# Finished outputs of a convolution and two FFN layers: turned on DVE in 32x32 blocks and stored in runs of 128 bytes, instead of turned on PE

## The chip, the cores and the metric

The kernel runs on one core of a Trainium2 chip. The metric is the device time of one execution, in microseconds; lower is better. The engines are PE (TensorE, matrix products), DVE (VectorE), ACT (ScalarE), POOL (GpSimd) and SP (SyncE, which here only issues DMAs). They run side by side and wait for each other through semaphores.

## What is computed

```python
# x [2, 4096, 192]; weight_gen [2, 4096, 8 heads, 7 taps]
w = softmax(weight_gen, axis=-1)
x_pad = six rows of zeros ahead of x          # a causal window of 7 tokens
out[b, s, h, :] = sum_k w[b, s, h, k] * x_pad[b, s + k, h, :]     # 24 channels per head
x = out.reshape(8192, 192)
h = x @ w_in;   g = np.maximum(0.01 * h, h);  x = g @ w_out       # 192 -> 2048 -> 192
h = x @ w_in2;  r = np.maximum(h, 0.0);       return (r * r) @ w_out2
```

All of it is in float32. Each product is made from a high and a low part of both operands ("hi" and "lo"), as three matmuls.

## The kernel before

The 8192 tokens are split into 16 chunks (`NCH`) of 512 tokens: partition p holds tokens 64p to 64p + 63, and a chunk is 4 of these per partition (`TPC`). A chunk passes two layers, so there are 32 segments (`SEGS`): segment s works on one layer (`LAYER[s]`) of one chunk (`CHUNK[s]`). The layers alternate: segments 0 and 1 are layer 0 (of chunks 0 and 1), then even segments are layer 1 and odd ones layer 0, and 30 and 31 are both layer 1. In the steady part one period is an even segment and an odd one.

A segment has 8 steps (`PR`). On PE, `up(s, j)` multiplies 256 of the 2048 hidden rows into one of two PSUM pairs (`hb`, "h_pair" in the profile), and `down(s, j)` multiplies the activated result into the accumulators `ym` and `yr`. Between them ACT and DVE make the high and low part of the activation: in layer 0 ACT writes both the high part and `g` from PSUM and DVE subtracts (`gate_lo`, writes "g_lo"); in layer 1 ACT writes `u`, DVE `g` (`gate_of`), ACT the high part (`gate_hi`), and DVE the low part. `down` runs about two steps behind `up`; `steps_of` writes the order out by hand: for a segment up 0, the last two downs of the segment before around up 1, then up 2, up 3, down 0, up 4, down 1, up 5, down 2, a turn, down 3, up 6, down 4, up 7, down 5. (In segments 0 and 2 the turn stands later.) No engine reorders anything: each works through its own list and waits for semaphores.

`up` and the turns take the two PSUM pairs by turns (`made`, `PAIR`), and each waits until the one two before it has been read (`pair_free`).

PE holds activations channel by token, while the input and output rows are token by channel. So there is a turn in each segment: before an odd segment `turn_x` transposes the next chunk's convolution, and in an odd segment s of 3 to 31 `turn_y` transposes the outputs of layer 1 that the segment before has finished. Those outputs take this way: ACT copies half of the accumulators (`fold` on ACT), DVE adds the other half (`fold`, at j = 1, and `fold_end`, at j = 2) into `y_main` (128 channels) and `y_rest` (the other 64), both in the tile "raw_w_in"; PE turns them with 12 transposes against an identity into a PSUM pair; ACT copies them from there into `y_tok` (`y_out`, at j = 5); SP stores `y_tok` with one DMA (`store`). DVE also does the convolution for the next chunk in slices between its other work (`conv_ops`, `IN_UP`, `IN_DOWN`). SP's list in the steady part is: wait for the convolution, load the next x window and tap logits, wait for the finished outputs, store. The very last chunk has its own end (`last_out`, `last_fold`, `last_turn`), which writes the same `y_tok` after it has waited for the stores of all earlier chunks.

Of the kernel before, what the change touches and what calls it, by code (L numbers as in the profile page):

```python
# [5 lines left out]
def conv_two_ffn_kernel(nc, x, wgen, w_in1, w_out1, w_in2, w_out2, out):  # L6
    fp32 = mybir.dt.float32
    fp32r = mybir.dt.float32r
    ALU = mybir.AluOpType
# [7 lines left out]
    P = 128  # L17
# [35 lines left out]


    NEXT_X = [CHUNK[s + 1] if s + 1 < SEGS and LAYER[s + 1] == 0 else None for s in range(SEGS)]
    Y_OUT = [CHUNK[s - 1] if s and LAYER[s - 1] == 1 else None for s in range(SEGS)]
    assert not any(a is not None and b is not None for a, b in zip(NEXT_X, Y_OUT))

    LATE_TURNS = (0, 2)

    def steps_of(s):


        turn = [("turn", s)] if NEXT_X[s] is not None or Y_OUT[s] is not None else []
        early, late = ([], turn) if s in LATE_TURNS else (turn, [])
        if s == 0:
            return ([("up", 0), ("up", 1), ("up", 2), ("down", 0), ("up", 3), ("down", 1), ("up", 4), ("down", 2), ("up", 5)]
                    + early + [("down", 3), ("up", 6), ("down", 4)] + late + [("up", 7), ("down", 5)])
        before = [[("down", -2)], [("down", -1)]]
# [14 lines left out]
    PAIR[("last turn",)] = len(made) % 2  # L84
    made.append(("last turn",))
    TURNS = [m for m in made if m[0] != "up"]

    SOFT = 6
    TAPS = 2 * K - 1
# [23 lines left out]
    with ctx:  # L113
# [55 lines left out]
        y_tok = raw_in[1][:, :, :].rearrange("p a c -> p (a c)").rearrange("p (t d) -> p t d", d=D)  # L169
        ident = sb("identity", [P, HP])  # L170


# [47 lines left out]
        y_free = sem("y_banks_free")  # L220
        y_summed = sem("y_rest_summed")
        y_taken = sem("y_taken")
        y_turned = sem("y_transposed")
        turned_taken = sem("transposed_pair_taken")

        last_rest_done = sem("last_y_rest_done")
# [13 lines left out]
        def _(sync):  # L240
# [56 lines left out]

            def store(c):

                if c < NCH - 1:  # L300
                    sync.wait_ge(turned_taken, TURNS.index(("turn", c * 2 + 3 if c < NCH - 2 else SEGS - 1)) + 1)
                else:
                    sync.wait_ge(last_out_act, 2)
                    sync.wait_ge(last_out_dve, 1)
# [21 lines left out]
            for c in range(NCH):  # L326
                if c + 3 < NCH:

                    sync.wait_ge(conv_op, before(c + 3))
                    load_chunk(c + 3)  # L330
                store(c)
            sync.wait_ge(stored, 16 * NCH)

        @block.gpsimd
        def _(pool):
# [13 lines left out]
        def _(act):  # L349
# [60 lines left out]
                act.activation(fold_main[:, :], ym[0][:, :], ACT.Copy).then_inc(half_out, 1)  # L410
                act.activation(fold_rest[:, :], yr[0][:, :], ACT.Copy).then_inc(half_out, 1)

            def y_out(c, pair):
                act.wait_ge(y_turned, c + 1)
                if c:

                    act.wait_ge(stored, 16 * c)
                act.activation(y_tok[:, :, 0:P].rearrange("p t (a d) -> p a t d", a=2),
                               hb[pair][:, :, 0:QC].rearrange("p a (t d) -> p a t d", d=HP), ACT.Copy)
                act.activation(y_tok[:, :, P:D].rearrange("p (a t) d -> p a t d", a=2),  # L420
                               hb[pair][:, :, QC:QC + P].rearrange("p a (t d) -> p a t d", d=REST),
                               ACT.Copy).then_inc(turned_taken, 1)

            def up_out(s, j):
                n = s * PR + j
                pair = PAIR[("up", n)]
# [26 lines left out]
            def last_out():  # L453
                act.wait_ge(last_rest_done, 1)
                act.activation(fold_rest[:, :], yr[0][:, :], ACT.Copy).then_inc(last_rest_copied, 1)
                act.wait_ge(down_done, SEGS * PR)
                act.activation(fold_main[:, :], ym[0][:, :], ACT.Copy).then_inc(last_main_copied, 1)

                act.wait_ge(stored, 16 * (NCH - 1))
# [3 lines left out]
                act.wait_ge(y_turned, NCH)  # L463
                act.activation(y_tok[:, :, 0:HP], hb[PAIR[("last turn",)]][:, 0, 0:QC].rearrange("p (t d) -> p t d", d=HP),
                               ACT.Copy).then_inc(last_out_act, 1)

            def segment(s):
                for j in range(PR):
# [39 lines left out]
                    if NEXT_X[s] is not None and j == (6 if s in LATE_TURNS else 5):  # L508
# [4 lines left out]
                    if Y_OUT[s] is not None and j == 5:  # L513
                        y_out(Y_OUT[s], PAIR[("turn", s)])
# [21 lines left out]
        def _(dve):  # L536
# [153 lines left out]
            def fold(s):  # L690
                dve.wait_ge(half_out, s * 2 + 1)

                if LAYER[:s + 2].count(1):
                    dve.wait_ge(staged_taken, LAYER[:s + 2].count(1))
                if LAYER[s] == 0:
                    dve.tensor_tensor(stage[:, :], ym[1][:, :], fold_main[:, :], ALU.add)
                else:

                    dve.tensor_tensor(y_main[:, :].rearrange("p (t a c) -> p a t c", a=2, c=HP),  # L699
                                      *(t.rearrange("p (a t c) -> p a t c", a=2, c=HP)  # L700
                                        for t in (ym[1][:, :], fold_main[:, :])), ALU.add)
                dve.wait_ge(half_out, s * 2 + 2)
                upper = fold_rest[REST:P, :]
                dve.tensor_tensor(fold_sum[:, :], yr[1][0:REST, :], fold_rest[0:REST, :], ALU.add).then_inc(y_summed, 1)  # L704
                dve.tensor_tensor(upper, yr[1][REST:P, :], upper, ALU.add).then_inc(y_free, 1)  # L705

            def fold_end(s):
# [3 lines left out]
                if LAYER[s] == 0:  # L711
                    dve.tensor_tensor(stage_rest[:, :], fold_sum[:, :], upper, ALU.add).then_inc(y_taken, 1)
                else:
                    one, two = (t.rearrange("p (a h t c) -> p h a t c", a=2, h=2, c=HP) for t in (fold_sum[:, :], upper))
                    for h in range(2):
                        last = dve.tensor_tensor(
                            y_rest[h * REST:(h + 1) * REST, :].rearrange("p (t a c) -> p a t c", a=2, c=HP),
                            one[:, h, :, :, :], two[:, h, :, :, :], ALU.add)
                    last.then_inc(y_taken, 1)

            def gate_of(s, j):
                n = s * PR + j
# [58 lines left out]
            def last_fold():  # L781
# [10 lines left out]
                dve.wait_ge(stored, 16 * (NCH - 1))  # L792
                dve.wait_ge(y_turned, NCH)
                dve.tensor_copy(y_tok[:, :, HP:P], hb[PAIR[("last turn",)]][:, 1, 0:QC].rearrange("p (t d) -> p t d", d=HP)
                                ).then_inc(last_out_dve, 1)

            def segment(s):
                for j in range(PR):
# [5 lines left out]
                        fold(s - 1)  # L804
                    if s and j == 2:
                        fold_end(s - 1)
                    if s == 0 and j == 5:
                        first_segment(j)
                    if s == 1:
# [62 lines left out]
        def _(pe):  # L872
# [59 lines left out]
                                            conv_rest[r, t, :, :].rearrange("p h d -> p (h d)"), ident[r, :])  # L932
                last.then_inc(x_turned, 1)

            def turn_y(s, key):

                pe.wait_ge(y_taken, s + 1)
                pair_free(key)
                h = hb[PAIR[key]]
                for t in range(TPC):  # L940
                    for i, r in enumerate(ROWS):
                        pe.transpose(h[:, i, t * HP:(t + 1) * HP], y_main[r, t * P:(t + 1) * P], ident[r, :])  # L942
                for t in range(TPC // 2):
# [101 lines left out]
            def last_turn():  # L1045
# [18 lines left out]
                last.then_inc(y_turned, 1)  # L1064

            turn_first()
            for s in range(SEGS):
                for what, j in steps_of(s):
# [8 lines left out]
                            down(s, j)  # L1077
                    elif s == 0:
                        turn_second(("turn", s))
                    elif NEXT_X[s] is not None:  # L1080
                        turn_x(NEXT_X[s], ("turn", s))
                    else:
                        turn_y(s - 1, ("turn", s))
            down(SEGS - 1, PR - 2)
            last_down()
            last_turn()
# [20 lines left out]
```

## Time and profile before

| | |
|---|---|
| median of 3 runs | 1139.68 us (1139.62 to 1139.77) |
| profiled execution | 1142.64 us |
| its span in the trace | 1140.9 us |
| PE busy | 1132.4 us (99%), granted clock 1.0 throughout |
| DVE busy | 854.9 us (75%) |
| ACT busy | 667.4 us (59%) |
| hardware DMA queue | 15280 packets, 30.14 MB |

The profile is of one execution. Its span runs from the first to the last instruction; the time of the execution includes what lies around it. Busy times are the time in which an engine had at least one instruction under way. In the trace a matmul's line is that of the helper that issues it: L963 is `up`, L1008 and L1012 are `down`, L942 and L945 `turn_y`, L928 and L931 `turn_x`.

### The profile page before, as it was taken

To read this page: it belongs to the slowest core of one execution; us is meant where nothing else is said; L and a number is where in the kernel's file an instruction comes from. 1 tells how busy PE (TensorE), PEld (TensorE's weight loads), DVE (VectorE), ACT (ScalarE), POOL (GpSimd) and SP (SyncE) were. 2 spreads that over 40 slices of the span, in tenths; PEclk is the share of its full clock that TensorE was granted. 3 is DMA by queue.
4 is the path that set the end of the run, shared out by engine and by line. 5 is a ranking of instruction groups with operands and counts; after the bars stand their busy time and mean duration, and the time that the engine had idled before them with its cause. 6 is when DMAs were issued, how large, how long until landed. Compare 5 with 4: busy or idle time off the path is not lost.

```text
span 1140.9 us, 22894 instructions
## 1 busy us (share of the span) xinstructions
PE 1132.4 (99%) x10276; PEld 1115.3 (98%) x10276; DVE 854.9 (75%) x1036; ACT 667.4 (59%) x815; POOL 3.8 (0%) x11
## 2 busy tenths in 40 slices
PE   8999999999999999999999999999999999999998
PEld 6899999999999999999999999999999999999998
DVE  7888776877768787687877878777687776874574
ACT  4665656566565665656556556555656656566564
POOL 1000000000000000000000000000000000000000
PEclk9999999999999999999999999999999999999999
DMA  7311001010000101001010010100101001000000
GB/s 176 107 57 40 1 15 40 15 40 13 8 35 15 40 15 40 1 15 40 15 40 1 15 40 15 40 1 15 40 15 40 1 15 40 15 1 15 1 1 28
DMA packets 15378, 31.60 MB, mean 28 GB/s; under 512 B 1590, under 2 KB 10932, under 8 KB 15280
## 3 DMA queue, kind: packets, MB, share of 16 engines
q1 hardware_dynamic: 15280, 30.14, 8.2%
q8 instruction: 80, 1.31, 0.5%
q14 instruction: 18, 0.15, 0.0%
HBM read 23.84 MB, written 6.29 MB: 26 GB/s over the span
## 4 chain that ended last, share of the span: by engine, by line
PE 96%; DVE 1%; DMA 1%; ACT 1%; SPq 0%; issue 0%; DVEq 0%
PE h_pair L963 45%; PE y_main_psum L1008 30%; PE y_rest_psum L1012 20%; DMA x_window<-in_x_dram 1%; DVE tap_product L577 0%; PE h_pair L942 0%; PE h_pair L928 0%; PE h_pair L897 0%; DMA raw_w_in<-in_moe_w_in_dram 0%; DVE g_lo L737 0%; SPq L284 0%; DVE u L614 0%; ACT g_hi L429 0%; ACT g L433 0%; ACT w_in_parts L353 0%
## 5 line engine op out<-in xcount | busy, mean ns | idle before, releaser
L963 PE MATMUL h_pair<-x_parts,w_in_parts 64*128 64x512 f32 x4590 | 568.3, 386 | 0.5 <-issue 0.4
L963 PEld LDWEIGHTS h_pair<-x_parts,w_in_parts 64*128 64x128 f32 x4590 | 518.1, 184 | 5.9 <-issue 0.8
L1008 PE MATMUL y_main_psum<-g_hi,w_out_parts 64*128 64x512 f32 x2040 | 451.3, 389 | 0.0
L737 DVE TENSOR_TENSOR g_lo<-g,g_hi 128x1024 fp32r<-128x1024 f32 x255 | 311.5, 1222 | 141.0 <-ACT g_hi L441 87.0
L1008 PEld LDWEIGHTS y_main_psum<-g_hi,w_out_parts 64*128 64x128 f32 x2040 | 242.6, 184 | 2.1 <-issue 0.2
L441 ACT ACTIVATE g_hi<-g 128x1024 fp32r<-128x1024 f32 x127 | 134.8, 1062 | 170.6 <-DVE g L728 170.6
L429 ACT ACTIVATE g_hi<-h_pair 128x1024 fp32r<-128x1024 f32 x128 | 131.7, 1029 | 175.5 <-PE h_pair L963 175.4
L1012 PE MATMUL y_rest_psum<-g_lo,w_out_parts 64*128 64x512 f32 x1020 | 224.6, 387 | 0.0
L1012 PE MATMUL y_rest_psum<-g_hi,w_out_parts 64*128 64x512 f32 x1020 | 224.3, 386 | 0.0
L1008 PE MATMUL y_main_psum<-g_lo,w_out_parts 64*128 64x512 f32 x1020 | 224.2, 386 | 0.0
L728 DVE SCALAR_TENSOR_TENSOR g<-h_pair,u 128x1024 f32<-128x1024 f32 x127 | 155.1, 1221 | 57.7 <-ACT u L435 57.2
L435 ACT ACTIVATE u<-h_pair 128x1024 f32<-128x1024 f32 x127 | 129.7, 1021 | 62.8 <-PE h_pair L963 62.4
L433 ACT ACTIVATE g<-h_pair 128x1024 f32<-128x1024 f32 x128 | 130.9, 1022 | 0.0
L1012 PEld LDWEIGHTS y_rest_psum<-g_hi,w_out_parts 64*128 64x128 f32 x1020 | 121.3, 184 | 0.9
L1008 PEld LDWEIGHTS y_main_psum<-g_lo,w_out_parts 64*128 64x128 f32 x1020 | 121.2, 184 | 0.9
L1012 PEld LDWEIGHTS y_rest_psum<-g_lo,w_out_parts 64*128 64x128 f32 x1020 | 121.2, 184 | 0.9
L577 DVE TENSOR_TENSOR tap_product<-x_window,tap_weights 128x768 f32<-128x768 f32 x91 | 85.2, 950 | 1.7 <-DMA x_window<-in_x_dram 1.7
L633 DVE TENSOR_TENSOR conv_out<-conv_out,tap_product 128x768 f32<-128x768 f32 x70 | 66.5, 950 | 0.5
L699 DVE TENSOR_TENSOR raw_w_in<-y_main_psum,x_window 128x512 f32<-128x512 f32 x15 | 10.4, 692 | 56.7 <-ACT x_window L410 56.7
L410 ACT ACTIVATE x_window<-y_main_psum 128x512 f32<-128x512 f32 x31 | 18.5, 598 | 24.7 <-PE y_rest_psum L1012 24.7
L705 DVE TENSOR_TENSOR x_window<-y_rest_psum,x_window 64x512 f32<-64x512 f32 x31 | 21.5, 694 | 1.0
L704 DVE TENSOR_TENSOR x_window<-y_rest_psum,x_window 64x512 f32<-64x512 f32 x31 | 21.2, 684 | 0.4
(107 smaller groups left out, 469.5 us busy)
## 6 DMA issues: line engine op xcount, KB each, us to landing
x_window<-in_x_dram SPq DMA_DIRECT2D x14, 960.0 KB, 4.6
out_dram<-raw_w_in SPq DMA_DIRECT2D x16, 384.0 KB, 2.3
raw_w_out<-in_moe_w_out_dram SPq DMA_DIRECT2D x16, 192.0 KB, 3.1
tap_logits<-in_weight_gen_dram SPq DMA_DIRECT2D x16, 112.0 KB, 4.6
raw_w_in<-in_moe_w_in_dram SPq DMA_DIRECT2D x8, 192.0 KB, 4.1
raw_w_in<-in_moe_w_in_dram SPq DMA_DIRECT2D x24, 64.0 KB, 3.2
x_window<-in_x_dram SPq DMA_DIRECT2D x1, 768.0 KB
x_window<-in_x_dram SPq DMA_DIRECT2D x4, 141.8 KB
```

The costliest lines, as they stand in the source:

```text
L429: act.activation(GH[n % 4][:, :, :], hb[pair][:, :, :], ACT.Prelu, alpha=0.01).then_inc(ghi_ready, 1)
L433: act.activation(gate[n % 2][:, :, :], hb[pair][:, :, :], ACT.Prelu, alpha=0.01).then_inc(g_ready, 1)
L435: act.activation(unit[:, :, :], hb[pair][:, :, :], ACT.Relu).then_inc(u_ready, 1)
L441: act.activation(GH[n % 4][:, :, :], gate[n % 2][:, :, :], ACT.Copy).then_inc(ghi_ready, 1)
L577: return dve.tensor_tensor(dst.rearrange("p (a g) -> p a g", g=G), xwin[slot][:, t * D:(t + TPC) * D].rearrange("p (a g) -> p a g", g=G), ...
L633: op = dve.tensor_tensor(total, total, prod[TAP_OPS[i - SOFT][1] % 2][:, :], ALU.add)
L705: dve.tensor_tensor(upper, yr[1][REST:P, :], upper, ALU.add).then_inc(y_free, 1)
L728: dve.scalar_tensor_tensor(gate[n % 2][:, :, :], hb[PAIR[("up", n)]][:, :, :], 0.0, unit[:, :, :], ALU.max, ALU.mult).then_inc(g_ready, 1)
L737: dve.tensor_tensor(GL[n % 4][:, :, :], gate[n % 2][:, :, :], GH[n % 4][:, :, :].bitcast(fp32), ALU.subtract).then_inc(glo_ready, 1)
L963: last = pe.matmul(h[:, i, :], w[r, slot, a, c], v[r, slot, b, :], start=first, stop=end)
L1008: return pe.matmul(ym[rows][:, :], w[r, c], g[r, i, :], start=start, stop=stop)
L1012: return pe.matmul(yr[rows][:, :], w[r, P:2 * P], g[r, i, :], start=start, stop=stop)
```

## The change

The outputs of layer 1 are no longer turned on PE. `turn_y` and ACT's `y_out` are gone; `fold` and `fold_end` write `y_main` and `y_rest` in the order in which PE left them. A new function on DVE, `blocks`, runs at j = 3 of the segment, ahead of that step's slice of convolution and of its `gate_lo`. It transposes the tile in blocks of 32 channels by 32 partitions' tokens, so that each partition then holds runs of 32 channels of a token. `store` writes these runs with 24 DMAs per chunk, each of 32 partitions x 4 tokens x 32 channels, that is 128 runs of 128 bytes. The last chunk keeps its own way (`store_last` is the old store), and the counts that wait for stores are changed to match.

```diff
-    Y_OUT = [CHUNK[s - 1] if s and LAYER[s - 1] == 1 else None for s in range(SEGS)]
...
-        turn = [("turn", s)] if NEXT_X[s] is not None or Y_OUT[s] is not None else []
+        turn = [("turn", s)] if NEXT_X[s] is not None else []
...
+    BL = 32
+    STORED = 16 * (P // BL) * (D // BL)
...
             def store(c):
-                if c < NCH - 1:
-                    sync.wait_ge(turned_taken, TURNS.index(("turn", c * 2 + 3 if c < NCH - 2 else SEGS - 1)) + 1)
...
+                sync.wait_ge(y_turned, c + 1)
+                first = c * TPC * D
+                for q in range(P // BL):
+                    for g in range(P // BL):
+                        sync.dma_start(bass.AP(out.tensor, first + g * BL * TPP * D + q * BL, [[TPP * D, BL], [D, TPC], [1, BL]]),
+                                       y_blocks[q * BL:(q + 1) * BL, g * P:(g + 1) * P].rearrange("p (t d) -> p t d", d=BL)
+                                       ).then_inc(stored, 16)
+                for g in range(P // BL):
+                    for q in range(REST // BL):
+                        a, h = g // 2, g % 2
+                        p = a * HP + q * BL
+                        sync.dma_start(bass.AP(out.tensor, first + g * BL * TPP * D + P + q * BL, [[TPP * D, BL], [D, TPC], [1, BL]]),
+                                       y_blocks[p:p + BL, NC + h * P:NC + (h + 1) * P].rearrange("p (t d) -> p t d", d=BL)
+                                       ).then_inc(stored, 16)
...
-            def y_out(c, pair):
-                act.wait_ge(y_turned, c + 1)
-                if c:
-
-                    act.wait_ge(stored, 16 * c)
-                act.activation(y_tok[:, :, 0:P].rearrange("p t (a d) -> p a t d", a=2),
-                               hb[pair][:, :, 0:QC].rearrange("p a (t d) -> p a t d", d=HP), ACT.Copy)
-                act.activation(y_tok[:, :, P:D].rearrange("p (a t) d -> p a t d", a=2),
-                               hb[pair][:, :, QC:QC + P].rearrange("p a (t d) -> p a t d", d=REST),
-                               ACT.Copy).then_inc(turned_taken, 1)
...
+            def blocks(c, s):
+                dve.wait_ge(y_taken, s + 1)
+                if c:
+                    dve.wait_ge(stored, STORED * c)
+                dve.transpose(y_blocks[:, 0:NC].rearrange("p (a h t d) -> p a t h d", a=2, t=TPC, d=BL), y_main[:, :])
+                dve.transpose(y_blocks[:, NC:NC + QC].rearrange("p (h t d) -> p t h d", t=TPC, d=BL),
+                              y_rest[:, :]).then_inc(y_turned, 1)
...
                     if s and j == 2:
                         fold_end(s - 1)
+                    if s and LAYER[s - 1] == 1 and j == 3:
+                        blocks(CHUNK[s - 1], s - 1)
...
-            def turn_y(s, key):
-
-                pe.wait_ge(y_taken, s + 1)
-                pair_free(key)
-                h = hb[PAIR[key]]
-                for t in range(TPC):
-                    for i, r in enumerate(ROWS):
-                        pe.transpose(h[:, i, t * HP:(t + 1) * HP], y_main[r, t * P:(t + 1) * P], ident[r, :])
-                for t in range(TPC // 2):
-                    for i, r in enumerate(ROWS):
-                        last = pe.transpose(h[:, i, QC + t * HP:QC + (t + 1) * HP], y_rest[r, t * P:(t + 1) * P],
-                                            ident[r, :])
-                last.then_inc(y_turned, 1)
```

How the lists of three engines change, in segment 3 (the first with a finished chunk). First PE, between `down(3, 2)`, whose last products are the first rows, and `down(3, 3)`. Before:

```order
L1008 MATMUL y_main_psum<-g_hi,w_out_parts 128x512 x2
L1008 MATMUL y_main_psum<-g_lo,w_out_parts 128x512 x2
L1012 MATMUL y_rest_psum<-g_lo,w_out_parts 128x512 x2
L942 MATMUL h_pair<-identity,raw_w_in 128x64 [waits g_ready,y_taken]
L942 MATMUL h_pair<-identity,raw_w_in 128x64 x7
L945 MATMUL h_pair<-identity,raw_w_in 128x64 x4
L1008 MATMUL y_main_psum<-g_hi,w_out_parts 128x512 [waits g_lo_ready]
```

And of the change (L1012 and L1016 are `down` there):

```order
L1012 MATMUL y_main_psum<-g_hi,w_out_parts 128x512 x2
L1012 MATMUL y_main_psum<-g_lo,w_out_parts 128x512 x2
L1016 MATMUL y_rest_psum<-g_lo,w_out_parts 128x512 x2
L1012 MATMUL y_main_psum<-g_hi,w_out_parts 128x512 [waits g_lo_ready]
L1012 MATMUL y_main_psum<-g_hi,w_out_parts 128x512
```

The 12 transposes and their two waits are gone, and `down(3, 3)`, with its wait for the low part of `g`, follows `down(3, 2)` at once.

Second DVE, from `fold_end` at j = 2 to `gate_lo(3, 3)`. Before:

```order
L716 TENSOR_TENSOR raw_w_in<-x_window 64x2x2x64
L567 TENSOR_REDUCE tap_sum<-tap_exp 128x32 [waits tap_exp_done,conv_op]
L569 TENSOR_SCALAR tap_denominator<-tap_sum 128x32 [waits conv_op]
L571 RECIPROCAL tap_reciprocal<-tap_denominator 128x32 [waits conv_op]
L572 TENSOR_TENSOR tap_weights<-tap_exp,tap_reciprocal 128x224 [waits conv_op]
L577 TENSOR_TENSOR conv_out<-x_window,tap_weights 128x768 [waits x_transposed,conv_op]
L737 TENSOR_TENSOR g_lo<-g,g_hi 128x1024 [waits g_ready]
L577 TENSOR_TENSOR tap_product<-x_window,tap_weights 128x768 [waits conv_op] x2
L633 TENSOR_TENSOR conv_out<-conv_out,tap_product 128x768 [waits conv_op]
L737 TENSOR_TENSOR g_lo<-g,g_hi 128x1024 [waits g_ready]
```

Of the change, the part from `gate_lo(3, 2)` on, with a row of the softmax ahead of it:

```order
L588 TENSOR_TENSOR conv_out<-x_window,tap_weights 128x768 [waits x_transposed,conv_op]
L753 TENSOR_TENSOR g_lo<-g,g_hi 128x1024 [waits g_ready]
L733 STREAM_TRANSPOSE raw_w_in<-raw_w_in 128x2x4x2x32 [waits stored,y_taken]
L734 STREAM_TRANSPOSE raw_w_in<-raw_w_in 128x4x2x32
L588 TENSOR_TENSOR tap_product<-x_window,tap_weights 128x768 [waits conv_op] x2
L644 TENSOR_TENSOR conv_out<-conv_out,tap_product 128x768 [waits conv_op]
L753 TENSOR_TENSOR g_lo<-g,g_hi 128x1024 [waits g_ready]
```

Two transposes stand between `gate_lo(3, 2)` and three operations of the convolution, behind which `gate_lo(3, 3)` waits its turn.

Third SP, one round of its steady list. Before:

```order
L269 DMA x_window<-in_x_dram 128x1920 [waits conv_op]
L272 DMA tap_logits<-in_weight_gen_dram 128x224
L305 DMA out_dram<-raw_w_in 128x768 [waits transposed_pair_taken]
L269 DMA x_window<-in_x_dram 128x1920 [waits conv_op]
L272 DMA tap_logits<-in_weight_gen_dram 128x224
```

Of the change:

```order
L275 DMA x_window<-in_x_dram 128x1920 [waits conv_op]
L278 DMA tap_logits<-in_weight_gen_dram 128x224
L311 DMA out_dram<-raw_w_in 32x4x32 [waits y_blocks_transposed]
L311 DMA out_dram<-raw_w_in 32x4x32 x15
L318 DMA out_dram<-raw_w_in 32x4x32 x8
L275 DMA x_window<-in_x_dram 128x1920 [waits conv_op]
```

One store becomes 24, behind a wait for DVE instead of one for ACT, and ahead of the next load.

## Rows read from the trace of the kernel before

**Rows 1.** The page: busy time by engine, and shares of the chain that ended last

```profile
PE 1132.4 (99%) x10276; PEld 1115.3 (98%) x10276; DVE 854.9 (75%) x1036; ACT 667.4 (59%) x815; POOL 3.8 (0%) x11
...
PE 96%; DVE 1%; DMA 1%; ACT 1%; SPq 0%; issue 0%; DVEq 0%
```

**Rows 2.** Windows: stretch, its length, busy PE, PEld, DVE, ACT, POOL, clock

```profile
145.12:214.95 69.83, 69.83 (x634) 69.75 (x633) 52.96 (x65) 40.96 (x51) 0.00 (x0) 1.00 0.07 23
```

**Rows 3.** Groups by line: `turn_y` on PE and `y_out` on ACT

```profile
L418 ACT ACTIVATE raw_w_in<-h_pair 128x512 f32<-128x512 f32 x15 | 9.0, 599 | 9.8 <-PE h_pair L945 9.8
...
L942 PE MATMUL h_pair<-identity,raw_w_in 64*128 64x64 f32 x120 | 6.9, 220 | 0.0
...
L420 ACT ACTIVATE raw_w_in<-h_pair 128x256 f32<-128x256 f32 x15 | 5.7, 379 | 0.0
...
L945 PE MATMUL h_pair<-identity,raw_w_in 64*128 64x64 f32 x60 | 5.1, 223 | 0.0
```

**Rows 4.** Timeline of PE, 205 to 220 us: start, us, line

```profile
207.92 2.26 PE L963 MATMUL h_pair<-x_parts,w_in_parts 64*128 64x512 f32 x18
209.96 0.44 PE L1008 MATMUL y_main_psum<-g_hi,w_out_parts 64*128 64x512 f32 x2
...
212.23 0.46 PE L942 MATMUL h_pair<-identity,raw_w_in 64*128 64x64 f32 x8
...
214.95 2.26 PE L963 MATMUL h_pair<-x_parts,w_in_parts 64*128 64x512 f32 x18
...
219.26 1.12 PE L963 MATMUL h_pair<-x_parts,w_in_parts 64*128 64x512 f32 x8
```

**Rows 5.** Groups by line: plain operations of DVE, mean ns of one behind the bar

```profile
L677 DVE CAST x_parts<-x_parts 64x512 fp32r<-64x512 f32 x30 | 12.7, 423 | 0.4
...
L639 DVE TENSOR_TENSOR conv_out<-conv_out,tap_product 128x512 f32<-128x512 f32 x14 | 9.6, 684 | 0.0
...
L636 DVE TENSOR_TENSOR conv_rest<-conv_out,tap_product 128x256 f32<-128x256 f32 x14 | 5.8, 414 | 0.0
```

**Rows 6.** Timeline of DVE, 205 to 224 us

```profile
205.90 1.82 DVE L577 TENSOR_TENSOR tap_product<-x_window,tap_weights 128x768 f32<-128x768 f32 x2
...
208.51 1.22 DVE L737 TENSOR_TENSOR g_lo<-g,g_hi 128x1024 fp32r<-128x1024 f32 x1
...
211.38 1.22 DVE L737 TENSOR_TENSOR g_lo<-g,g_hi 128x1024 fp32r<-128x1024 f32 x1
...
215.46 1.21 DVE L737 TENSOR_TENSOR g_lo<-g,g_hi 128x1024 fp32r<-128x1024 f32 x1
...
217.59 0.42 DVE L687 CAST x_parts<-x_parts 64x512 fp32r<-64x512 f32 x1
...
223.53 1.23 DVE L737 TENSOR_TENSOR g_lo<-g,g_hi 128x1024 fp32r<-128x1024 f32 x1 [1.66 <-ACT g L433]
```

**Rows 7.** Timeline of ACT: `g` of step 5 of segment 3

```profile
211.14 1.02 ACT L433 ACTIVATE g<-h_pair 128x1024 f32<-128x1024 f32 x1
```

**Rows 8.** SP: issue times in ns (min/median/max), landing, and the next load

```profile
L284 SPq DMA_DIRECT2D raw_w_in<-in_moe_w_in_dram x24: 596/597/1469, 3.9 to 72.1; - x24
...
L305 SPq DMA_DIRECT2D out_dram<-raw_w_in x16: 332/343/348, 143.9 to 1138.2; - x16
...
DMA to landing us min/median/max: 2.3/2.3/2.4
...
242.14 0.33 SPq L269 DMA_DIRECT2D x_window<-in_x_dram  x1
```

**Rows 9.** DMA: packets, MB, share of 16 engines; 213 to 217, then 76 to 90 us

```profile
q1 hardware_dynamic: 144, 0.39, 24.4%
...
q1 hardware_dynamic: 544, 0.39, 9.4%
```

**Rows 10.** Timelines of DVE and ACT in the last segment

```profile
1112.41 1.22 DVE L728 SCALAR_TENSOR_TENSOR g<-h_pair,u 128x1024 f32<-128x1024 f32 x1
...
1136.82 0.38 ACT L461 ACTIVATE raw_w_in<-h_pair 128x256 f32<-128x256 f32 x1 [0.49 <-PE h_pair L1057]
```

More of the change, by code:

```diff
@@ L55, in conv_two_ffn_kernel @@
     NEXT_X = [CHUNK[s + 1] if s + 1 < SEGS and LAYER[s + 1] == 0 else None for s in range(SEGS)]
-    Y_OUT = [CHUNK[s - 1] if s and LAYER[s - 1] == 1 else None for s in range(SEGS)]
-    assert not any(a is not None and b is not None for a, b in zip(NEXT_X, Y_OUT))
     LATE_TURNS = (0, 2)
     def steps_of(s):
-        turn = [("turn", s)] if NEXT_X[s] is not None or Y_OUT[s] is not None else []
+        turn = [("turn", s)] if NEXT_X[s] is not None else []
         early, late = ([], turn) if s in LATE_TURNS else (turn, [])
@@ L168, in conv_two_ffn_kernel @@
         y_rest = raw_in[0][:, 2, :]
-        y_tok = raw_in[1][:, :, :].rearrange("p a c -> p (a c)").rearrange("p (t d) -> p t d", d=D)
+        y_blocks = raw_in[1][:, :, :].rearrange("p a c -> p (a c)")
+        y_tok = y_blocks.rearrange("p (t d) -> p t d", d=D)
         ident = sb("identity", [P, HP])
@@ L222, in conv_two_ffn_kernel @@
         y_taken = sem("y_taken")
-        y_turned = sem("y_transposed")
+        y_turned = sem("y_blocks_transposed")
+        last_main_turned = sem("last_y_main_transposed")
         turned_taken = sem("transposed_pair_taken")
@@ L298, in store, with store_last @@
             def store(c):
-                if c < NCH - 1:
-                    sync.wait_ge(turned_taken, TURNS.index(("turn", c * 2 + 3 if c < NCH - 2 else SEGS - 1)) + 1)
-                else:
-                    sync.wait_ge(last_out_act, 2)
-                    sync.wait_ge(last_out_dve, 1)
+                sync.wait_ge(y_turned, c + 1)
[12 more added lines that the diff above has]
+                                       ).then_inc(stored, 16)
+            def store_last(c):
+                sync.wait_ge(last_out_act, 2)
+                sync.wait_ge(last_out_dve, 1)
                 sync.dma_start(out_rows[:, c * (TPC * D):(c + 1) * (TPC * D)],
@@ L330, in _ @@
                     load_chunk(c + 3)
-                store(c)
-            sync.wait_ge(stored, 16 * NCH)
+                if c + 1 < NCH:
+                    store(c)
+                else:
+                    store_last(c)
+            sync.wait_ge(stored, STORED * (NCH - 1) + 16)
         @block.gpsimd
@@ L457, in last_out @@
                 act.activation(fold_main[:, :], ym[0][:, :], ACT.Copy).then_inc(last_main_copied, 1)
-                act.wait_ge(stored, 16 * (NCH - 1))
+                act.wait_ge(stored, STORED * (NCH - 1))
                 act.wait_ge(last_rest_turned, 1)
@@ L512, in segment @@
                         spread_hi_rest(s + 1)
-                    if Y_OUT[s] is not None and j == 5:
-                        y_out(Y_OUT[s], PAIR[("turn", s)])
                     if s + 1 < SEGS and LAYER[s + 1] == 1 and j == 4:
@@ L697, in fold @@
                 else:
-                    dve.tensor_tensor(y_main[:, :].rearrange("p (t a c) -> p a t c", a=2, c=HP),
-                                      *(t.rearrange("p (a t c) -> p a t c", a=2, c=HP)
-                                        for t in (ym[1][:, :], fold_main[:, :])), ALU.add)
+                    dve.tensor_tensor(y_main[:, :], ym[1][:, :], fold_main[:, :], ALU.add)
                 dve.wait_ge(half_out, s * 2 + 2)
@@ L713, in fold_end @@
                 else:
[L714 to L718, printed above, removed]
-                    last.then_inc(y_taken, 1)
+                    for a in range(2):
+                        last = dve.tensor_tensor(y_rest[a * HP:(a + 1) * HP, :], fold_sum[:, a * QC:(a + 1) * QC],
+                                                 upper[:, a * QC:(a + 1) * QC], ALU.add)
+                    last.then_inc(y_taken, 1)
+            def blocks(c, s):
[5 more added lines that the diff above has]
+                              y_rest[:, :]).then_inc(y_turned, 1)
             def gate_of(s, j):
@@ L790, in last_fold @@
                                   by_t(fold_main[:, :]), ALU.add).then_inc(y_taken, 1)
-                dve.wait_ge(stored, 16 * (NCH - 1))
-                dve.wait_ge(y_turned, NCH)
+                dve.wait_ge(stored, STORED * (NCH - 1))
+                dve.wait_ge(last_main_turned, 1)
                 dve.tensor_copy(y_tok[:, :, HP:P], hb[PAIR[("last turn",)]][:, 1, 0:QC].rearrange("p (t d) -> p t d", d=HP)
@@ L1063, in last_turn @@
                         last = pe.transpose(h[:, i, t * HP:(t + 1) * HP], y_main[r, t * P:(t + 1) * P], ident[r, :])
-                last.then_inc(y_turned, 1)
+                last.then_inc(last_main_turned, 1)
             turn_first()
@@ L1079, in _ @@
                         turn_second(("turn", s))
-                    elif NEXT_X[s] is not None:
+                    else:
                         turn_x(NEXT_X[s], ("turn", s))
-                    else:
-                        turn_y(s - 1, ("turn", s))
             down(SEGS - 1, PR - 2)
```

2 lines of the change are left out of this document (1 added, 1 removed).

## Prediction

> **What bounds the kernel now.** I read four views, in this order. The page first: PE (TensorE) is busy for 1132.4 of 1140.9 us, DVE (VectorE) for 75% and ACT (ScalarE) for 59% of the span, and the chain that ended last is 96% PE [rows 1]. Then the busy time of one full period of the steady part, two segments long, one of each layer: in 69.83 us PE is busy for 69.83, DVE for 52.96, ACT for 40.96 [rows 2]. So PE doesn't wait for anybody there: whatever is taken from PE's stream shortens the period, as long as no one else becomes late. Then the groups by line for what the edit touches, and last the timelines of PE, DVE and ACT around one turn of finished outputs (segment 3, near 212 us), to see who would be late next.
>
> **What is removed from PE.** In `turn_y`, 12 transposes for each of 15 chunks, 180 in all: 120 at L942 and 60 at L945, 220 ns each, with overlap [rows 3]. What they cost on PE is not their summed time but how far they push the next `up` apart. In rows 4, `up(3,5)` starts at 207.92 and its `down(2)` at 209.96, so an `up` holds PE for 2.04 us. `up(3,6)` starts at 214.95 and `up(3,7)` at 219.26: an `up` and a `down` take 4.31, so a `down` takes 2.27. Between 207.92 and 214.95 lie one `up`, two `down`s and the turn: 7.03 - 2.04 - 2 x 2.27 = 0.45 us for the turn, its switch of weights and refill included. Check against the period: 69.83 - 16 x 4.31 = 0.87 for one turn of x (kept) and one of y, 0.44 each. So 15 x 0.45 = 6.75 us leave PE's path. All other matmuls keep their order; the pair of PSUM banks that the turn held goes to the next `up`, which then waits for the `up` two before it, a looser condition than before. Nothing there is late: cost 0.
>
> **What is removed from ACT.** `y_out`: 599 + 379 ns per chunk [rows 3]. ACT is busy for 59%, so this gives nothing by itself.
>
> **What is added on DVE.** Two transposes per chunk, 128x512 and 128x256, both from SBUF to SBUF, ahead of the convolution's work and `gate_lo` of j = 3. `fold` and `fold_end` only write in another order, with the same element counts: 0. No transpose stands in this trace on DVE, so the price has to be bounded. From below: a copy of 64x512 takes 423 ns [rows 5], and the smaller one can't be below nothing, so 0.42 us for the pair. The nearest rows are the ordinary two-operand ones, 684 ns for 128x512 and 414 ns for 128x256 [rows 5], 1.1 us for the pair; (684 - 414) / 256 = 1.05 ns for each element and 0.14 us fixed. From above I take four passes over each element, as for an engine that moved 32-bit data a byte at a time: 4 x 768 x 1.05 + 2 x 0.14 = 3.5 us. I take 1.1 us: a transpose in blocks streams as many elements per partition as those rows, and nothing in the trace makes a plain SBUF operation of DVE dearer per element. The Trainium skill, "Vector Engine (DVE) Microarchitecture Reference", section 3.8, says the 32x32 array sustains one element per cycle and lane; no run here shows it yet, and by it the sum would stay as it is.
>
> Who waits behind these two on DVE? First `gate_lo(3,3)`, which starts at 208.51 and takes 1.22, done at 209.73 [rows 6]. PE wants it for `down(3,3)`, which now follows `down(3,2)` at 212.23, where the turn stood [rows 4]. That leaves 2.50 us of cover; 1.1 fits with 1.4 to spare. Without cover each us would cost 14 us in all. Second, ACT reuses the buffer of `g`: its `g` of j = 5 starts at 211.14 [rows 7] and needs that same `gate_lo`, then done at 210.83; it just fits, and were it late, `up(3,7)` at 219.26 - 0.45 is the first to notice, 6 us later. Third, DVE's later pieces move by the same 1.1: `gate_lo(3,4)` ends at 212.60 + 1.1 against `down(3,4)` at 214.95 + 2.04 - 0.45 = 216.54; `gate_lo(3,5)` ends at 216.67 + 1.1 against `down(3,5)` at 219.26 + 2.04 - 0.45 = 220.85; the last spread of x's low part ends at 218.01 + 1.1 against the next segment's first `up` at 219.26 + 4.31 - 0.45 = 223.12 [rows 4, 6]. All keep 2.8 us or more. Then DVE stands idle for 1.66 us ahead of 223.53 [rows 6], which swallows the shift. Segments after chunk 12 have no convolution on DVE and more room. In the last segment the pair goes between `g` of j = 3, done at 1113.63, and its `gate_lo` [rows 10], inside the wait for ACT's `g_hi`. DVE's load per period becomes 52.96 + 1.1 of 69.4 us: it doesn't become the bound.
>
> **What changes for the stores.** Instead of one DMA of 128 rows of 3072 bytes, 24 DMAs per chunk, each 128 runs of 128 bytes: 3072 runs, 192 per DMA engine. Issuing on SP's queue: 343 ns for the old store, 597 ns for the dearest plain load of 64 rows (1469 once) [rows 8]; with about 0.04 between issues, 24 take 9.2 to 15.3 us. Moving: 544 packets, 512 of them of 768 bytes, took 9.4% of 16 engines in 14 us, 39 ns each; the old store's 144 packets took 24.4% of 16 engines in 4 us, 108 ns each [rows 9]. A run of 128 bytes is nearest to the smaller: 192 x 39 = 7.5 us, hidden under the issues; by the dear one 20.7 us. I take 39. Landing adds 2.3 [rows 8]. A store is thus down some 12 to 18 us after DVE's transposes, by the dear packet 23.
>
> Who waits for it? SP's next work is the load of the next x window at 242.14 [rows 8]; the new stores begin when DVE's pair ends, at 205.90 + 1.1 = 207.0 [rows 6], and are issued by 223, so that load keeps its time, and the next `blocks` comes 69 us later. Only chunk 14 is pressing: DVE and ACT wait for all stores before they write the last chunk into the same buffer. Its transposes end at 1113.63 + 1.1 = 1114.7; ACT's first write stood at 1136.82 [rows 10], now 0.45 earlier: 21.6 us of cover. By my prices the store lands 4 to 10 us before that.
>
> **The sum.** The profiled execution took 1142.64 us with a span of 1140.9, the median of the three runs shown is 1139.68: the profile's own run is 3.0 us above it, and I carry the difference over, not the level. -6.75 (PE) + 0 (DVE, covered) + 0 (stores, covered) = -6.75: span 1134.2, and 1139.68 - 6.75 = **1132.9 us**.
>
> **Rivals.** (1) DVE's transposes are slow and `gate_lo(3,3)` holds PE up. This is the one on the slower side. It starts to cost at 2.50 us for the pair and eats the whole gain at 2.50 + 6.75 / 14 = 2.98. At the upper price of 3.5 it is 14 x 1.0 - 6.75 = +7.3: 1147 us. For it speaks that DVE has no idle time behind the pair until 223.53 - 1.66 = 221.87 [rows 6], so that every tenth is passed on; against it that DVE's rows for plain operations follow 1.05 ns per element [rows 5]. Chance 7%, of which 2% between 1135 and 1137.
>
> (2) The store of chunk 14 is late. It decides from (21.6 - 2.3) / 192 = 100 ns per run, or 0.80 us per DMA issued; at 136 ns per run, or 1.1 us per issue, the gain is gone. With the dear packet of 108 ns it is 1.4 us late: 1134.3. If each short run cost twice that packet, 216 ns, it would land 22.2 us late: 1155. For it speaks that the runs are six times shorter than any data packet here, so that the fixed part of a packet is not in a row; against it that going from 108 to 39 ns the packets do get cheaper with size. Chance 9%, half of it on each side of no gain. The Trainium skill, "DMA: Bandwidth & Descriptors", section Specifications, says that below 512 bytes a transfer does a read-modify-write; no run here shows one. Doubling the 39 ns packet gives 15 us, still under the cover, doubling the 108 ns one gives this rival's 1155; that rule is why I give it 9% and not less.
>
> (3) The edit takes work from PE but PE finds another wait, so nothing is gained: within 0.2% of 1139.7. The places checked above are those where DVE or ACT feed PE next, and the nearest has 1.4 us left for 0.45 gained. Chance 4%.
>
> **How the numbers follow.** Forecast: 80%. Its own range is 1132 to 1134, from 0.44 to 0.47 us per turn and a tail of a few tenths. To hold 8 in 10 with the partial cases of (1) and (2) I give 1131.5 to 1136. No change can be told within 0.2%, 2.3 us. Faster by more: 80 + 2 + 5 = 87%; same: 4%; slower: 9%.
>
> **What the changed profile would show.** PE's distance from `up(3,5)` to `up(3,6)` at 6.58 us and a period of 69.38; two transposes on DVE of about 0.7 and 0.4 us; no wait of PE for `gate_lo`; ACT without the two copies; 24 issues per chunk on SP, and the last of chunk 14 landed before about 1136. The forecast is wrong if DVE's pair is above 2.5 us, if SP needs over 0.8 us per issue, or if PE's busy time falls and its idle time grows as much.

## The result and the profile after

The changed kernel takes 1132.52 us (median of 6 runs, 1132.39 to 1133.39) against 1139.68: the ratio is 0.9937, with a 95% interval of 0.9924 to 0.995. That is 7.2 us less; 1132.9 was forecast. The profiled execution took 1133.32 us, with a span of 1131.5.

The page's busy times, the shares of its chain, and its row for the short stores:

```profile
PE 1125.0 (99%) x10096; PEld 1103.0 (97%) x10096; DVE 868.8 (77%) x1066; ACT 654.5 (58%) x785; POOL 3.8 (0%) x11
...
PE 97%; DVE 1%; ACT 1%; SPq 0%; DMA 0%; issue 0%; DVEq 0%
...
out_dram<-raw_w_in SPq DMA_DIRECT2D x360, 16.0 KB, 1.5
```

PE lost 180 matmuls and 7.4 us of busy time against [rows 1], DVE gained 30 instructions and 13.9 us, ACT lost 30 and 12.9. The chain is PE's, as before.

One period of the steady part in windows, from one `up(s, 6)` to the same two segments on (columns as in [rows 2]):

```profile
142.25:211.62 69.37, 69.37 (x622) 69.33 (x621) 53.90 (x67) 40.09 (x48) 0.00 (x0) 1.00 0.08 22
```

69.37 us instead of 69.83, and PE still busy for all of it: 0.46 less per period, and nothing waited for.

PE's timeline at the place of [rows 4]:

```profile
205.05 2.26 PE L967 MATMUL h_pair<-x_parts,w_in_parts 64*128 64x512 f32 x18
...
211.62 2.26 PE L967 MATMUL h_pair<-x_parts,w_in_parts 64*128 64x512 f32 x18
...
215.93 2.26 PE L967 MATMUL h_pair<-x_parts,w_in_parts 64*128 64x512 f32 x18
```

From `up 5` to `up 6` it is 6.57 us; it was 7.03. The next step, 4.31, is what it was.

DVE's timeline at the place of [rows 6]:

```profile
201.89 1.22 DVE L753 TENSOR_TENSOR g_lo<-g,g_hi 128x1024 fp32r<-128x1024 f32 x1
203.03 0.71 DVE L733 STREAM_TRANSPOSE raw_w_in<-raw_w_in 128x512 f32<-128x512 f32 x1
203.66 0.40 DVE L734 STREAM_TRANSPOSE raw_w_in<-raw_w_in 128x256 f32<-128x256 f32 x1
203.98 1.79 DVE L588 TENSOR_TENSOR tap_product<-x_window,tap_weights 128x768 f32<-128x768 f32 x2
...
206.55 1.22 DVE L753 TENSOR_TENSOR g_lo<-g,g_hi 128x1024 fp32r<-128x1024 f32 x1
...
220.19 1.23 DVE L753 TENSOR_TENSOR g_lo<-g,g_hi 128x1024 fp32r<-128x1024 f32 x1 [0.27 <-ACT g L446]
```

The two transposes last 0.71 and 0.40 us, about as long as plain operations of their sizes (0.68 and 0.41) [rows 5], but the pair occupies only 203.03 to 203.98, 0.95 us, since the next operation starts before the last has ended. `gate_lo` of j = 3 ends at 206.55 + 1.22 = 207.77, and PE wants it at 205.05 + 2.04 + 2.27 = 209.36: 1.59 us of cover are left. Further on, the wait of 1.66 us shrinks to 0.27, by 1.39: about the pair's 0.95 and the 0.46 that PE no longer takes.

SP's timeline, one round of the steady part and the end:

```profile
204.09 8.54 SPq L311 DMA_DIRECT2D out_dram<-raw_w_in  x16
212.67 3.76 SPq L318 DMA_DIRECT2D out_dram<-raw_w_in  x8
238.81 0.36 SPq L275 DMA_DIRECT2D x_window<-in_x_dram  x1
...
1105.71 7.44 SPq L311 DMA_DIRECT2D out_dram<-raw_w_in  x16
1113.20 3.75 SPq L318 DMA_DIRECT2D out_dram<-raw_w_in  x8
```

And ACT's first write of the last chunk into the stored tile:

```profile
1127.46 0.39 ACT L474 ACTIVATE raw_w_in<-h_pair 128x256 f32<-128x256 f32 x1 [0.50 <-PE h_pair L1061]
```

The store of chunk 14 is issued in 11.24 us, 0.47 for each DMA. By the median of 1.5 us from issue to landing its last piece lands at about 1118.4, 9 us before ACT needs the tile. No store was issued faster: the one at 204.09 took 12.34 us, and single issues varied (median 0.43 us, the longest 1.73). The DMA engines in the 30 us from 205 on, nearly all of them one chunk's short runs (packets, MB, share of 16 engines):

```profile
q1 hardware_dynamic: 3415, 0.39, 8.2%
```

That is 0.082 x 16 x 30 / 3415 = 11.5 ns for each packet, the small ones that signal completion included.

The spans of the two profiled executions differ by 9.4 us, more than the medians. Part of that is not the change. Here is PE's first product, the first `up`, in the profiled execution of before, and then of after:

```profile
15.75 2.80 PE L972 MATMUL h_pair<-x_parts,w_in_parts 64*128 64x512 f32 x18 [0.17 <-ACT x_parts L369]
```

```profile
13.29 2.80 PE L976 MATMUL h_pair<-x_parts,w_in_parts 64*128 64x512 f32 x18 [0.17 <-ACT x_parts L393]
```

The profiled execution of before began its first product 2.46 us later; ahead of it PE had waited 0.50 and 1.45 us for results of the first convolution, which it did not in the other. From `up 5` of the turn at [rows 4] to the end, with 14 turns to come, it is 1140.9 - 207.92 = 932.98 us before and 1131.5 - 205.05 = 926.45 after: 6.53 us for 14 turns, 0.466 each, 7.0 for 15. And 7.0 + 2.46 is the 9.4.

### The profile page after: what moved, and what is told of

Its sections match the earlier page's. It is cut to its first block, busy times and chain, and to the rows that moved or that the text cites. A ratio compares the mean times of both kernels' runs of the same rounds, so it can differ in the third digit from the quotient of the medians.

```text
span 1131.5 us, 22864 instructions
## 1 busy us (share of the span) xinstructions
PE 1125.0 (99%) x10096; PEld 1103.0 (97%) x10096; DVE 868.8 (77%) x1066; ACT 654.5 (58%) x785; POOL 3.8 (0%) x11
## 4 chain that ended last, share of the span: by engine, by line
PE 97%; DVE 1%; ACT 1%; SPq 0%; DMA 0%; issue 0%; DVEq 0%
PE h_pair L967 45%; PE y_main_psum L1012 30%; PE y_rest_psum L1016 20%; PE y_rest_psum L908 1%; PE h_pair L946 0%; PE h_pair L915 0%; DVE g_lo L753 0%; DMA raw_w_in<-in_moe_w_in_dram 0%; DVE tap_product L588 0%; SPq L290 0%; DVE u L625 0%; ACT g_hi L442 0%; ACT g L446 0%; PE y_main_psum L915 0%; ACT w_in_parts L377 0%
## 5 line engine op out<-in xcount | busy, mean ns | idle before, releaser
L1012 PE MATMUL y_main_psum<-g_hi,w_out_parts 64*128 64x512 f32 x2040 | 448.6, 387 | 0.0
L1012 PEld LDWEIGHTS y_main_psum<-g_hi,w_out_parts 64*128 64x128 f32 x2040 | 241.2, 184 | 3.4 <-issue 0.3
L1016 PE MATMUL y_rest_psum<-g_lo,w_out_parts 64*128 64x512 f32 x1020 | 223.7, 386 | 0.0
L1016 PE MATMUL y_rest_psum<-g_hi,w_out_parts 64*128 64x512 f32 x1020 | 223.6, 386 | 0.0
L1012 PE MATMUL y_main_psum<-g_lo,w_out_parts 64*128 64x512 f32 x1020 | 223.6, 386 | 0.0
L1016 PEld LDWEIGHTS y_rest_psum<-g_hi,w_out_parts 64*128 64x128 f32 x1020 | 120.6, 184 | 1.6
L1012 PEld LDWEIGHTS y_main_psum<-g_lo,w_out_parts 64*128 64x128 f32 x1020 | 120.6, 184 | 1.6
L1016 PEld LDWEIGHTS y_rest_psum<-g_lo,w_out_parts 64*128 64x128 f32 x1020 | 120.6, 184 | 1.6
```

The lines of the kernel that those rows point to most:

```text
L1012: return pe.matmul(ym[rows][:, :], w[r, c], g[r, i, :], start=start, stop=stop)
L1016: return pe.matmul(yr[rows][:, :], w[r, P:2 * P], g[r, i, :], start=start, stop=stop)
```

## The experiments

The theory to be tested: PE's 12 transposes per chunk are the whole gain, and DVE's pair and the short stores are covered. The rivals are those of the prediction, and one more: that the removal is worth more than 7 us and part of it is given back. Each experiment ran beside the kernel before on its chip; its medians there were 1139.98 (the first four) and 1139.95 (the last three).

**Only the removal.** Edit to the changed kernel (the 24 DMAs of `store` go, one takes their place):

```diff
-    STORED = 16 * (P // BL) * (D // BL)
+    STORED = 16
...
-                sync.wait_ge(y_turned, c + 1)
...
+                sync.wait_ge(y_taken, 2 * c + 3)
+                sync.dma_start(out_rows[:, c * (TPC * D):(c + 1) * (TPC * D)],
+                               y_tok[:, :, :].rearrange("p t d -> p (t d)")).then_inc(stored, 16)
...
-                    if s and LAYER[s - 1] == 1 and j == 3:
-                        blocks(CHUNK[s - 1], s - 1)
```

> The turn and ACT's copies are gone, but DVE doesn't transpose and the store stays one DMA of 128 rows; what it stores for chunks 0 to 14 is whatever the tile holds, so the outputs of these chunks are left out. Theory (PE's 12 transposes are the whole gain, DVE's pair and the short stores are covered): 6.9 us below the kernel before, 1132.6, the same as the changed kernel within 0.5 us. Rival (DVE's pair or the stores cost something that the larger removal hides): below the changed kernel by what they cost, 1 us or more.

Measured: 1132.65 us (6 runs), ratio to before 0.9934 (0.9922 to 0.9946). The changed kernel's ratio is 0.9937. Without DVE's pair and without the short stores it is no faster. The interval alone would let 1.4 us pass; the table behind the last experiment narrows that to 0.1.

**PE's turn put back, unread.** Edit to the changed kernel (the turn has the 12 transposes of `turn_y`, and waits for the same things; nothing waits for it to be read):

```diff
+        if s and LAYER[s - 1] == 1:
+            turn = [("unread turn", s)]
...
+            def unread_turn(s, key):
+                pe.wait_ge(y_taken, s + 1)
+                pair_free(key)
+                h = hb[PAIR[key]]
+                for t in range(TPC):
+                    for i, r in enumerate(ROWS):
+                        pe.transpose(h[:, i, t * HP:(t + 1) * HP], y_main[r, t * P:(t + 1) * P], ident[r, :])
+                for t in range(TPC // 2):
+                    for i, r in enumerate(ROWS):
+                        pe.transpose(h[:, i, QC + t * HP:QC + (t + 1) * HP], y_rest[r, t * P:(t + 1) * P], ident[r, :])
```

> The changed kernel, with PE's 12 transposes of y put back at their old place into their old PSUM pair, and nobody reads them. DVE's pair and the 24 short stores stay. Theory: all of the gain is given back, 1139.5 within 0.5 us of the kernel before, and the distance from up 5 to up 6 is 7.03 us again. Rival (part of the gain came from ACT's removed copies or from looser waits): between 1133.5 and 1138.5.

Measured: 1140.08 us (12 runs), ratio 0.9999 (0.999 to 1.0007). PE's timeline at the same turn:

```profile
205.40 2.26 PE L983 MATMUL h_pair<-x_parts,w_in_parts 64*128 64x512 f32 x18
209.71 0.47 PE L964 MATMUL h_pair<-identity,raw_w_in 64*128 64x64 f32 x8
...
212.44 2.26 PE L983 MATMUL h_pair<-x_parts,w_in_parts 64*128 64x512 f32 x18
```

7.04 us from `up 5` to `up 6`, as before. All of the gain is given back although ACT's copies stay gone, so these are worth nothing; and DVE's pair together with the stores costs nothing here either.

**Only the short stores.** Edit to the kernel before (the counts of `stored` follow; the last chunk keeps its store):

```diff
-                sync.dma_start(out_rows[:, c * (TPC * D):(c + 1) * (TPC * D)],
-                               y_tok[:, :, :].rearrange("p t d -> p (t d)")).then_inc(stored, 16)
...
+                for g in range(4):
+                    for q in range(6):
+                        sync.dma_start(bass.AP(out.tensor, c * TPC * D + g * 32 * TPP * D + q * 32,
+                                               [[TPP * D, 32], [D, TPC], [1, 32]]),
+                                       y_tok[g * 32:(g + 1) * 32, :, q * 32:(q + 1) * 32]).then_inc(stored, 16)
```

> The kernel before, with PE's turn and ACT's copies as they were; only the store of chunks 0 to 14 is 24 DMAs of 128 runs of 128 bytes. Theory: no change, within 0.5 us of the kernel before, since a store is down some 13 us after its first issue and nobody waits for it sooner; only the store of chunk 14 is pressing, and it begins 8 us later here than in the changed kernel, at about 1122.5, so it should land at about 1135.2, 1.6 us ahead of the last chunk's first write at 1136.8. Rival (short runs are dear): the last chunk waits, 1 us or more is added.

Measured: 1139.95 us (12 runs), ratio 0.9997 (0.9989 to 1.0005). SP's timeline at the end, then ACT's first write of the last chunk:

```profile
1119.47 11.24 SPq L311 DMA_DIRECT2D out_dram<-raw_w_in  x24
1135.18 0.35 SPq L306 DMA_DIRECT2D out_dram<-raw_w_in  x1
```

```profile
1133.80 0.38 ACT L468 ACTIVATE raw_w_in<-h_pair 128x256 f32<-128x256 f32 x1 [0.50 <-PE h_pair L1064]
```

The issues end at 1130.71. By the median of 1.5 us the last piece lands at about 1132.2 (the slowest landing of this run took 3.4), and ACT starts at 1133.80 after the same 0.50 us of waiting for PE as ever: some 1.6 us to spare, as expected. In the kernel before this store would have been the tight one; DVE's transposes also bring it forward.

**The same runs in six DMAs.** Edit to the run above:

```diff
-                for g in range(4):
-                    for q in range(6):
...
+                for q in range(6):
+                    sync.dma_start(bass.AP(out.tensor, c * TPC * D + q * 32, [[TPP * D, P], [D, TPC], [1, 32]]),
+                                   y_tok[:, :, q * 32:(q + 1) * 32]).then_inc(stored, 16)
```

> As the run before, with the same runs of 128 bytes in 6 DMAs of 128 partitions instead of 24 of 32. If the time of a store is that of the issues on SP, about 0.47 us each, its six issues take some 3 us and all has landed 5 us after the first issue. If it is that of the runs on the DMA engines, it takes as long as before, 12 to 13 us.

Measured once: 1140.07 us. What it shows is in its trace. SP's timeline, then the stores' landing, then the DMA packets from 205 to 235 us:

```profile
211.18 3.15 SPq L310 DMA_DIRECT2D out_dram<-raw_w_in  x6
```

```profile
DMA to landing us min/median/max: 1.8/1.9/2.3
...
q1 hardware_dynamic: 3168, 0.39, 8.4%
```

A chunk is issued in 3.15 us and down about 5 us after the first issue. With 12.7 ns per packet (0.084 x 16 x 30 / 3168), 192 runs per DMA engine take 2.4 us. So it is the number of DMAs that makes the changed kernel's store last about 13 us, not the length of its runs.

**Two pairs of transposes on DVE.** Edit to the changed kernel, ahead of the pair that is stored (`raw_out` is free by then):

```diff
+                for i in range(1):
+                    e = raw_out[0][:, :, :, :].rearrange("p a j d -> p (a j d)")
...
+                    dve.transpose(e[:, 0:NC].rearrange("p (a h t d) -> p a t h d", a=2, t=TPC, d=BL), y_main[:, :])
+                    dve.transpose(e[:, NC:NC + QC].rearrange("p (h t d) -> p t h d", t=TPC, d=BL),
+                                  y_rest[:, :]).then_inc(extra_turned, 1)
```

> The changed kernel, with DVE's pair of transposes done twice, once into a tile that nobody reads. In the changed kernel gate_lo of j = 3 ends 1.59 us before PE wants it; the second pair takes 0.95 to 1.1 us. Theory of a cover: no change, within 0.5 us of the changed kernel. Rival (every us on DVE in the busy half of the segment shows): 13 segments with a convolution times 0.95 = 12 us more.

Measured: 1132.98 us (5 runs), ratio 0.9942 (0.993 to 0.9955). The interval takes in the changed kernel's 0.9937, and `up 5` and `up 6` stand at 204.63 and 211.21, 6.58 apart. DVE's `gate_lo` of j = 3:

```profile
207.06 1.22 DVE L762 TENSOR_TENSOR g_lo<-g,g_hi 128x1024 fp32r<-128x1024 f32 x1
```

It ends at 208.28, 0.66 us before 204.63 + 4.31 = 208.94. A second pair is covered too. ACT, though, now waits for `gate_lo` before it writes `g` of j = 5 (us in total, times, longest):

```profile
ACT g L447 <- DVE g_lo L762: 4.6, 13, 0.4
```

This is the second waiter of the prediction. In the changed kernel it never waits for `gate_lo`, which ends at 207.77 where that `g` starts at 208.26; here it waits in 13 segments, and PE notices nothing.

**Four pairs.** The same edit with three unread pairs, into `raw_out[0]`, `raw_out[1]` and `raw_out[0]`.

> The same with four pairs, three of them unread: 2.85 to 3.3 us more on DVE than in the changed kernel, ahead of gate_lo of j = 3. Theory: the cover of 1.59 us is used up and PE waits 1.26 to 1.7 us in down 3, in the 13 segments where DVE also has a slice of convolution there (the other two have more room): 16 to 22 us more, 1149 to 1155. Rival (PE doesn't wait for this, or DVE's time shows in full): 1132.5, or 13 x 2.85 = 37 us more.

Measured: 1150.62 us (4 runs), ratio 1.0095 (1.0081 to 1.0108), so 18 us above the changed kernel. PE's waits (us in total, times, longest), then its timeline:

```profile
PE y_main_psum L1021 <- DVE g_lo L762: 13.2, 13, 1.0
```

```profile
205.82 2.21 PE L976 MATMUL h_pair<-x_parts,w_in_parts 64*128 64x512 f32 x18
...
211.31 0.50 PE L1021 MATMUL y_main_psum<-g_hi,w_out_parts 64*128 64x512 f32 x2 [1.01 <-DVE g_lo L762]
...
213.74 2.21 PE L976 MATMUL h_pair<-x_parts,w_in_parts 64*128 64x512 f32 x18
```

PE waits 13 times, once in each segment whose j = 3 also holds a slice of convolution, and only for `gate_lo`. In the segment shown `up 6` comes 7.92 us after `up 5` instead of 6.57, and 1.35 x 13 = 17.6 of the 18. PE's own wait, 1.0 us, is below the 1.26 to 1.7 that was expected: `gate_lo` ends 5.43 us after `up 5` instead of 2.72, so three more pairs took 2.71 and not 2.85 or more. The total is inside what was expected all the same, since PE lost more than it waited (see the last section). This is the slower rival of the prediction, made real, at the place and with the mechanism named there.

**The store of chunk 14 twice.** Edit to the changed kernel (the last chunk waits for both):

```diff
                     store(c)
+                    if c == NCH - 2:
+                        sync.wait_ge(stored, STORED * (NCH - 1))
+                        store(c)
```

> The changed kernel, with the store of chunk 14 done a second time once the first has landed; the last chunk waits for both. In the changed kernel the issues take 11.2 us from 1105.7, the last lands 1.5 later, and the last chunk's first write is at 1127.46, so the cover is 21.75 us and 9.0 of it is unused. Two stores take 25.4 us. Theory: ACT's first write waits 3.7 us, the end comes 3.1 to 3.7 us later, 1135.6 to 1136.2. Rival (the stores aren't what the last chunk would wait for): no change.

Measured: 1137.01 us (7 runs, 1136.11 to 1139.11), ratio 0.9974 (0.9963 to 0.9985): 4.5 above the changed kernel in the medians, and 0.8 above the upper end of what was expected. SP's and ACT's timelines at the end:

```profile
1106.67 7.44 SPq L311 DMA_DIRECT2D out_dram<-raw_w_in  x16
1114.15 3.75 SPq L318 DMA_DIRECT2D out_dram<-raw_w_in  x8
1119.02 8.38 SPq L311 DMA_DIRECT2D out_dram<-raw_w_in  x16
1127.45 3.78 SPq L318 DMA_DIRECT2D out_dram<-raw_w_in  x8
```

```profile
1132.36 0.38 ACT L477 ACTIVATE raw_w_in<-h_pair 128x256 f32<-128x256 f32 x1 [4.44 <-DMA out_dram<-raw_w_in]
```

ACT waits 4.44 us for the stores, 3.94 more than for PE. From `up 5` at 206.04 to the end of the span, 1135.7, it is 929.66 us, 3.2 more than in the changed kernel and inside the 3.1 to 3.7 that was expected of the edit. The profiled execution also began 1.2 us later than the changed kernel's (first product at 14.52 us), which belongs to the start and not to the edit. The other six runs left no trace, so why the median is above the expected time isn't shown.

**All traces by one stretch.** From `up 5` of segment 5 to the end of the span, which leaves out the start (us):

| run | `up 5` | end | stretch |
|---|---|---|---|
| kernel before | 207.92 | 1140.9 | 932.98 |
| unread turn | 205.40 | 1138.4 | 933.00 |
| only the short stores | 204.94 | 1137.9 | 932.96 |
| the same runs in six DMAs | 205.38 | 1138.3 | 932.92 |
| changed kernel | 205.05 | 1131.5 | 926.45 |
| only the removal | 204.50 | 1130.9 | 926.40 |
| two pairs | 204.63 | 1131.1 | 926.47 |
| four pairs | 205.82 | 1148.4 | 942.58 |
| store of chunk 14 twice | 206.04 | 1135.7 | 929.66 |

The four with PE's transposes agree within 0.1 us, and so do the three without them whose cover holds; 6.5 us lie between the groups. DVE's pair, the copies on ACT and the short stores are therefore worth less than 0.1 us each in this stretch. The four pairs add 16.1 us there for the 12 waits that are left, 1.34 each.

## Why the prediction was right, point by point

**PE is the bound, and a turn costs 0.45 us.** Right. The turn measured 0.46 to 0.47; 15 x 0.45 = 6.75 was 0.2 to 0.3 us low against 15 x 0.466 = 7.0, since the sum rested on a few rounded starts, where 14 turns at once give 0.466. The medians differ by 7.2. Putting the turn back gave all back, and removing the turn and the copies, with nothing in their place, gave no more than the change.

**ACT's copies and the looser wait for the PSUM pair are worth nothing.** Right. With the copies still gone, the unread turn alone returns to 1140.08. That run doesn't test the looser wait, for its turn takes a PSUM pair again, and `up 6` then waits until `up 5` has been read, as in the kernel before. That the stricter wait cost nothing shows in the kernel before itself: PE is busy for all 69.83 us of the period [rows 2].

**DVE's pair at 1.1 us.** Right in its kind: 0.71 + 0.40 by duration, on DVE's path 0.95, between the bounds of 0.42 and 3.5 and near the value taken. The Trainium skill's one element per cycle and lane ("Vector Engine (DVE) Microarchitecture Reference", section 3.8) agrees with the trace as far as it can be seen. Behind another transpose, as the stored pair is in the runs with two and four pairs, the two last 669 and 402 ns in the mean, a difference of 267 ns for 256 elements: 1.04 ns each, where plain operations take 1.05 [rows 5]. Behind `gate_lo` the larger one lasts 705 ns in the mean. How long a cycle is, no run here shows.

**2.50 us of cover for `gate_lo` of j = 3.** Right: 0.91 of it was used and 1.59 is left. Two pairs were free, four cost 1.35 us in each of 13 segments. The second waiter, ACT's `g` of j = 5, was called rightly as well: it fits with 0.49 us left (the prediction had 0.31), and with two pairs, when it was late, PE didn't notice. The prediction counted 14 such segments for this rival; the last two of the 15 with a finished chunk have no slice of convolution there. It also called the segment of [rows 4], [rows 6] and [rows 7] segment 3. The first turn of y, in segment 3, stands at 142.40, so these rows are those of segment 5, one period on; all its times are taken from that one segment, and the sum doesn't change.

**The stores.** Right that nobody waits, and that the issues set the pace: they took 11.2 to 12.6 us per chunk, inside the forecast's 9.2 to 15.3. The price of a run was three times too high: 39 ns were taken, from packets of a load, and 12 measured. It sat behind the issues, so it didn't enter the sum. Rival (2) would have needed 100 ns per run or 0.80 us per DMA issued; 12 ns and 0.47 us are far from both. Its mechanism exists, as the store done twice shows.

**The rule against the change.** The Trainium skill, "DMA: Bandwidth & Descriptors", section Specifications, has transfers below 512 bytes do a read-modify-write. No run here shows what such a write does inside, but its time is seen: a run of 128 bytes takes a third of the 39 ns of a packet of 768. The measurement decides: the store in 24 DMAs was limited by its issues.

**Nothing was given back.** Rival (3) is out: the period is 0.46 us shorter, PE has no wait in it, and the removal alone gave no more than the whole change.

## What to carry to other kernels

When one engine is busy for all of a steady period, the price of an operation is how far it pushes its neighbours apart, read between two fixed rows, and the sum over periods comes out to a few tenths. Moving that operation to another engine is free as long as the first consumer behind it there keeps its cover: here 2.50 us, of which the move used 0.91, and past which each of 13 segments paid. To see differences below 1 us, compare traces over a stretch that leaves out the start. For stores in short runs, count the DMAs first and the runs second, and look for the one store with a deadline, which here is the last before the tile is written again.

## What the runs showed of the hardware

- A 128-byte run to memory took 12 ns of a DMA engine's time, in 24 DMAs of 128 runs or in 6 of 512. SP issued a DMA of 128 runs per 0.47 us, with single ones up to 1.73, and a DMA of 512 runs per 0.53 us.
- A transpose in 32x32 blocks of float32 on DVE takes as long as an ordinary operation of its size (0.67 to 0.71 us for 128x512), with strided output, and back to back a pair of 128x512 and 128x256 costs 0.91 to 0.96 us.
- Here a late operand cost PE more than its lateness: in the four pairs `gate_lo` ended at 211.25, 1.12 us after PE could have begun at 210.13, and `up 6` came 1.35 us late. PE began 0.06 us after `gate_lo` ended, and its products from there to `up 6` took 2.43 us instead of 2.27.
- The start varies by itself: in the profiled executions PE's first product came at 13.26 to 15.75 us, though no edit touched what comes ahead of it. With the same start the kernel before had it at 15.75, the two runs that only change its stores at 13.41 and 13.32, so single spans can differ by 2.4 us without any cause in the edit.
